# Another order of work around the chunk recurrence: the masking, the signs, the folds and tiles of the Fourier transform, and the first parts

## The reference

```python
# 1. complex recurrence per head (B=4, H=8, S=768, D=48)
scale = min(|a|, 0.999) / (|a| + 1e-6);  a_n = a * scale
for t in range(S):
    S_state = a_n[t] * S_state + outer(k[t], v[t])      # complex, k v real
    y[t]    = q[t] @ Re(S_state)
# 2. u = x + Re(FFT over channels(FFT over tokens(x))), x = y as (B, 768, 384)
#    un = layernorm(u);  x2 = u + relu(un @ w_ch1) @ w_ch2
# 3. token mixing and a second channel product on x2
```

## Time and profile before

| | us |
|---|---|
| median of 3 runs | 1131.13 (1129.0 to 1136.8) |
| the profiled execution, its own time | 1134.15 |
| its span | 1132.4 |
| TensorE busy in it | 1008.8 (89%) |
| VectorE busy | 538.2 (48%) |
| ScalarE busy | 341.4 (30%) |

### The profile page before, as it was taken

The page is one execution under the profiler, slowest core; times in us unless marked ns, Lnnn a source line. Parts: engine busy times, 40 slices in busy tenths (PEclk is TensorE's granted clock), DMA queues, the critical chain, the costliest instruction groups (busy, mean ns, idle before and its releaser), DMA issues. The chain is left out here.

```text
span 1132.4 us, 15567 instructions
## 1 busy us (share of the span) xinstructions
PE 1008.8 (89%) x6082; PEld 971.8 (86%) x6082; DVE 538.2 (48%) x1040; ACT 341.4 (30%) x515; POOL 29.9 (3%) x15
## 2 busy tenths in 40 slices
PE   0469799989969973999999999968999999999998
PEld 0348699979969863999999999968999999999998
DVE  6798877897973338332432422225223322331411
ACT  6636545655621113121122112124121220310310
POOL 0000000000000004000000000004000000000000
PEclk9859759779969895999999999999999999999999
DMA  4559777765757013602102101001001000100000
GB/s 151 150 152 301 221 226 224 208 196 156 196 145 281 22 44 100 223 29 84 33 22 69 42 28 63 15 23 43 15 8 46 24 14 21 42 21 15 6 22 21
DMA packets 96887, 104.79 MB, mean 93 GB/s; under 512 B 13121, under 2 KB 90433, under 8 KB 96834
## 3 DMA queue, kind: packets, MB, share of 16 engines
q1 hardware_dynamic: 96834, 104.07, 29.7%
HBM read 70.93 MB, written 33.11 MB: 92 GB/s over the span
## 5 line engine op out<-in xcount | busy, mean ns | idle before, releaser
L1125 ACT ACTIVATE hh<-mbank 128x384 fp32r<-128x384 f32 x192 | 94.5, 492 | 370.8 <-PE mbank L1309 370.8
L1218 DVE SCALAR_TENSOR_TENSOR hl<-mbank,hh 128x384 fp32r<-128x384 f32 x192 | 107.1, 558 | 200.9 <-ACT hh L1125 200.9
L1307 PE MATMUL mbank<-nTh,w1h 128*128 128x384 f32 x576 | 193.9, 337 | 0.7 <-DVE w1l L1240 0.7
L1308 PE MATMUL mbank<-nTl,w1h 128*128 128x384 f32 x576 | 193.2, 335 | 0.0
L1309 PE MATMUL mbank<-nTh,w1l 128*128 128x384 f32 x576 | 193.2, 335 | 0.0
L1307 PE MATMUL mbank<-w2h,hh 128*128 128x384 f32 x576 | 193.1, 335 | 0.0
L1309 PE MATMUL mbank<-w2h,hl 128*128 128x384 f32 x576 | 192.4, 334 | 0.0
L1308 PE MATMUL mbank<-w2l,hh 128*128 128x384 f32 x576 | 192.4, 334 | 0.0
L1307 PEld LDWEIGHTS mbank<-nTh,w1h 128*128 128x128 f32 x576 | 108.8, 189 | 1.5 <-issue 1.3
L1308 PEld LDWEIGHTS mbank<-nTl,w1h 128*128 128x128 f32 x576 | 108.8, 189 | 0.0
L1309 PEld LDWEIGHTS mbank<-nTh,w1l 128*128 128x128 f32 x576 | 108.7, 189 | 0.0
(11 more groups left out here) (152 smaller groups left out, 1320.7 us busy)
## 6 DMA issues: line engine op xcount, KB each, us to landing
kT<-k_turn SPq DMA_DIRECT2D x24, 384.0 KB, 3.6
qT<-q_turn SPq DMA_DIRECT2D x24, 384.0 KB, 4.4
q_turn<-w_raw SPq DMA_DIRECT2D x30, 192.0 KB, 4.4
k_turn<-t SPq DMA_DIRECT2D x24, 192.0 KB, 4.0
k_turn<-w_early SPq DMA_DIRECT2D x24, 192.0 KB, 4.6
u_scratch<-y_sb SPq DMA_DIRECT2D x24, 192.0 KB, 3.1
w_raw<-in_moe_w_ch SPq DMA_DIRECT2D x2, 2304.0 KB, 10.3
x_early<-u_scratch SPq DMA_DIRECT2D x4, 1152.0 KB, 10.0
```

Source lines behind the costliest of these rows:

```text
L1125: nc.scalar.activation(hh[:, m, :], mm_bank[(g * (KF + TPG) + m) % 2][:, 0:TG], ACT.Relu).then_inc(h_high, 1)
L1218: nc.vector.scalar_tensor_tensor(out=hl[:, m, :], in0=mm_bank[(g * (KF + TPG) + m) % 2][:, 0:TG], scalar=0.0, in1=hh[:, m, :].bitcast(fp32 ...
L1307: nc.tensor.matmul(out, lh, rh, start=(n == 0), stop=False)
L1308: nc.tensor.matmul(out, lh, rl, start=False, stop=False)
```

## The change

1. **Masking first.** `masked(m)` now stands right behind `advance_state(m-1)`, ahead of `add_transform`, folds, `phases` and `products`.
2. **Signs by ScalarE.** The two comparisons leave VectorE. `arctangents` gets two more operations of ScalarE on the whole part, Sign and Identity, and `half_angles` multiplies the arctangent by the sign. `t4` carries the offset.
3. **Products in pairs.** Chunk 0 of a part in stage 4, chunks 1 and 2 together in stage 5. SP turns chunk 0 a chunk earlier than the other two.
4. **Fourier work spread.** Before: fold, `middle` and all three widths at `j` = 1; sequence transforms 0; 1, 2; 3, 4; 5 at `j` = 2, 3, 4, 5. Now: fold 2, `middle`, width 2 at `j` = 0; folds and widths 1, 0 at `j` = 1; sequence transforms 0, 1; 2, 3; 4; 5. Tiles 0, 1 and 2, 3 are added in pairs over two banks (`f_pair`). At the very end `middle` and width 2 of block 3 stand ahead of the last `turn_y`.
5. **The smallest end** (`least`) is reduced once at the end, not per part.
6. **First parts.** `magnitudes(p0)` ahead of `squares(p1)`; the second chunk of part 1 is phased behind the products of part 0; on SP the loads for part 2 and part 3 stand ahead of `turn_decay(p0)`.
7. **ScalarE in a chunk.** `keys_turned` first, then arctangents or sines, then `evacuate_y(m-1)`, and only then squares, magnitudes or inverses and factors, then copies of widths, then `y_turned(m-1)`. Before, `evacuate_y` stood behind all of these stages.
8. `keep_busy` 3 to 4 per chunk of block 0, 6 to 5 at the start.

```diff
@@ tables of places
-            return {2: [0], 3: [1, 2], 4: [3, 4], 5: [5]}.get(j, [])
+            return {2: [0, 1], 3: [2, 3], 4: [4], 5: [5]}.get(j, [])
...
+            return [(n, i, tiles) for i, tiles in {3: [(0, 2)], 4: [(2, 2)], 5: [(4, 1)], 0: [(5, 1)]}.get(j, []) if n >= 0]
+
+        def widths_at(j):
+            return {0: [2], 1: [1, 0]}.get(j, [])
@@ SP, first parts and loop
             turn_over(0)
+            load_qk(p2)
+            load_gates(p3)
             turn_decay(p0)
-            load_gates(p3)
-            load_qk(p2)
...
                 if (m - 1, 4) in stage_at:
-                    p = stage_at[m - 1, 4]
-                    turn_over(p.first)
-                    turn_over(p.first + 1)
+                    turn_over(stage_at[m - 1, 4].first)
                 if (m - 1, 5) in stage_at:
+                    turn_over(stage_at[m - 1, 5].first + 1)
                     turn_over(stage_at[m - 1, 5].first + 2)
@@ ScalarE, arctangents and loop
+                A(im_b[p.r][:, :, T], re_b[p.r][:, :, T], ACT.Sign, scale=3.0,
+                  bias=nearly_zero[:, 0:1]).then_inc(act_step[s], 1)
+                act.wait_ge(act_step[s], act0[p.n] + 12)
+                A(t4[:, :, angles_room(p)], im_b[p.r][:, :, T], ACT.Identity, scale=-0.25,
+                  bias=quarter[:, 0:1]).then_inc(act_step[s], 1)
...
+                if j < NCH - 1:
+                    keys_turned(m)
                 if (m, 3) in stage_at:
                     arctangents(stage_at[m, 3])
                 if (m, 4) in stage_at:
                     sines(stage_at[m, 4])
-                if j < NCH - 1:
-                    keys_turned(m)
+                if m:
+                    evacuate_y(m - 1)
...
-                if m:
-                    evacuate_y(m - 1)
-                if (m, 2) in stage_at:
                     angle_tables()
-                if b and j == 1:
+                if b and j == 0:
                     middle(b - 1)
-                    for n in range(KD):
+                if b:
+                    for n in widths_at(j):
                         widths(b - 1, n)
@@ VectorE, loop
                     advance_state(m - 1)
-                for n, i in added_at(m):
-                    add_transform(n, i)
-                if b and j == 1:
-                    fold_sequence(b - 1)
+                masked(m)
+                for n, i, tiles in added_at(m):
+                    add_transform(n, i, tiles)
+                if b:
+                    for n in widths_at(j):
+                        fold_sequence(b - 1, n)
                 if (m, 3) in stage_at:
-                    phases(stage_at[m, 3])
+                    half_angles(stage_at[m, 3])
+                    phases(stage_at[m, 3], range(3))
                 if (m, 4) in stage_at:
-                    products(stage_at[m, 4], range(2))
+                    products(stage_at[m, 4], PAIRS[stage_at[m, 4].n][0:1])
                 if (m, 5) in stage_at:
-                    products(stage_at[m, 5], [2])
-                masked(m)
+                    products(stage_at[m, 5], PAIRS[stage_at[m, 5].n][1:2])
@@ TensorE, end
+            middle(B - 1)
+            width_transform(B - 1, 2)
             turn_y(NM - 1)
...
-            middle(B - 1)
-            for n in range(KD):
-                width_transform(B - 1, n)
+            width_transform(B - 1, 1)
+            width_transform(B - 1, 0)
```

More of the change, by code:

```diff
@@ L72, in recurrence_and_fourier @@
         stage_at = {(p.first - LEAD + k, k): p for p in parts[2:] for k in range(LEAD)}
-        GA = 14
-        GV = [12 + 5 * p.chunks for p in parts]
+        PAIRS = [[range(0, 1), range(1, 3)] if p.chunks == 3 else [range(p.chunks)] for p in parts]
+        GA = 16
+        GV = [10 + 3 * p.chunks + 2 * len(PAIRS[p.n]) for p in parts]
         act0 = [GA * p.turn for p in parts]
@@ L249, in _ @@
                     turn_decay(stage_at[m, 4])
-                for n, i in added_at(m - 1):
-                    store_u(n, i)
+                for n, i, tiles in added_at(m - 1):
+                    for tile in range(i, i + tiles):
+                        store_u(n, tile)
                 if m % 3 == 1:
@@ L511, in products @@
                 re, im = re_b[p.r], im_b[p.r]
-                dve.wait_ge(act_step[s], act0[p.n] + 14)
-                for i in chunks:
-                    T = slice(i * CT, (i + 1) * CT)
+                dve.wait_ge(act_step[s], act0[p.n] + 16)
+                for pair in chunks:
+                    i = pair.start
+                    T = slice(i * CT, pair.stop * CT)
                     dve.wait_ge(vec_step[s], products_done(p, i))
@@ L561, in add_transform @@
-            def add_transform(b, i):
-                n = b * NT + i
-                x = y_sb[:, n % YR, :]
-                dve.wait_ge(b_made, n + 1)
-                cc, sn = f_bank[i % 2][:, 0:FH], f_bank[i % 2][:, FH:2 * FH]
-                low, high = x[:, 0:FH], x[:, DM - 1:FH - 1:-1]
+                if n == 0:
+                    V.memset(fold[:, 1, :, 0:1], 0.0)
+                    V.tensor_copy(fold[:, 0, :, 0:1], yT[:, :, 0:1])
+                first, end = max(n * P, 1), (n + 1) * P
@@ new lines, in fold_sequence, with add_transform @@
+                fwd, back = yT[:, :, first:end], yT[:, :, S - first:S - end:-1]
+                V.tensor_tensor(fold[:, 0, :, first:end], fwd, back, ALU.add)
+                V.tensor_tensor(fold[:, 1, :, first:end], fwd, back, ALU.subtract).then_inc(folded, 1)
+            halves_added = []
+            def add_transform(b, i, tiles):
+                n, halves_done = b * NT + i, len(halves_added) + 1
+                halves_added.append(n)
+                x = y_sb[:, n % YR:n % YR + tiles, :]
+                dve.wait_ge(b_made, n + tiles)
+                f = f_pair[:, i % 2:i % 2 + tiles, :]
+                cc, sn = f[:, :, 0:FH], f[:, :, FH:2 * FH]
+                low, high = x[:, :, 0:FH], x[:, :, DM - 1:FH - 1:-1]
@@ L587, in _ @@
             scaled(p0)
+            logs(p1)
             ends(p1)
             tangents(p1)
-            phases(p0)
+            half_angles(p0)
+            phases(p0, range(1))
             scaled(p1)
-            phases(p1)
-            products(p0, range(1))
+            half_angles(p1)
+            phases(p1, range(1))
+            products(p0, PAIRS[0])
+            phases(p1, range(1, 2))
             squared(p2)
-            products(p1, range(2))
+            products(p1, PAIRS[1])
             logs(p2)
@@ L767, in _ @@
                     update(m)
-                if m < NCH:
-                    keep_busy(3)
                 if m == NCH:
                     pe.wait_ge(wide_tables_in, 5 * 16)
-                if b and j == 1:
+                if not b:
+                    keep_busy(4)
+                if b and j == 0:
                     middle(b - 1)
-                    for n in range(KD):
+                if b:
+                    for n in widths_at(j):
                         width_transform(b - 1, n)
-                if b:
                     for n in transformed_at(j):
```

144 lines of the change are left out of this document (68 added, 76 removed).

## The result

The changed kernel takes **1150.98 us** (median of 4 executions, 1150.66 to 1152.23) against 1131.91 (1129.0 to 1136.8) for the kernel before on the same chip: a ratio of 1.0166, interval 1.0129 to 1.0203. It is slower by 19 us, above the range of 1100 to 1138, where 1118.4 was forecast.

The account below looks back on a forecast made before the run. Block 0 bound by SP's queue, block 1 by a slow clock, block 2 by VectorE, block 3 by one long wait. Terms -2.0 - 0.7 + 0.9 - 7.8 - 3.1 = -12.7 gave 1118.4 us; range 1100 to 1138.

Parts of the forecast that it names:

- Six waits for additions: At `j` = 3 and 4, sequence transforms wait for paired additions behind masking: 1.4 us each, bounds 0 to 2.5.
- The wait for `yT` in chunks 12 and 18: Second half of `turn_keys` waits for ScalarE's late copy of `turn_y`: 2.8 us, once per block with preparation.
- the tail: From the last outputs to the first sequence transform: 13.5 us becomes 10.4, so -3.1; low clock may return (2 us).
- the start: Before chunk 6: 2.0 us gained, handed through SP's chain to turn 6, so -2.0; chunk 6 still waits for `kT`.
- two waits at `j` = 1: Behind sines, a table load and `magnitudes` on ScalarE, TensorE waits 2.0 us for `yT` in chunks 8 and 14.
- The wait for folds at `j` = 1: Fold late because VectorE comes from the phases of `j` = 0: 1.4 us, bounds 0 to 2.5.
- the term for the lower clock: Block 1 begins behind a wait at low clock: 6.5 us, 4.5 in its first chunk and 2 in the next.
- The sum of a block: 71 us of TensorE work plus waits gives 80.0 us: block 1 -0.7, block 2 +0.9, block 3 -7.8.
- block 1 bound by a slow clock: Chunks 6 to 11 of the kernel before: 87.2 us with TensorE at a mean clock of 0.76 of full.
- The prediction's own sign of being wrong: More than two stretches at the lower clock between chunk 8 and 418 us would show the forecast wrong.
- rival (c): ScalarE's four waits in `turn_keys` (blocks 1, 2) each bring lower clock, up to 6.5 us: +13, 1144 us; chance 0.13.

Follow-up runs that it names:

- additions first: The changed kernel with the additions of transformed tiles ahead of the masking again on VectorE: 1127.11 us, ratio 0.9932 to the kernel before.
- the filled kernel: The changed kernel with idle products of 384 columns where TensorE would wait, no wait removed: 1126.94 us, ratio 0.9943 to the kernel before.
- the second profile: The changed kernel run and profiled again, nothing altered: 1146.02 us, ratio 1.008 to the kernel before.
- both: The changed kernel with additions ahead of masking again and ScalarE's copy of the outputs back behind the stages: 1116.98 us, ratio 0.9822 to the kernel before.
- both, keys filled: The version with additions ahead of masking and the outputs' copy later, plus idle products in the key waits ahead of chunks 4 and 6: 1109.3 us, ratio 0.9775.

## Why the prediction was wrong, step by step

**Right: which waits would form, and how long.** Six waits for additions of 1.4 us were forecast ("a new wait of 1.4 us at `j` = 3, the same at `j` = 4"), and six of 1.44 to 1.45 came; a pair's additions take 2.0 us (190.09 to 192.17), as taken:

```profile
188.82 1.36 DVE L554 TENSOR_TENSOR pr<-bank,mask 128x512 f32<-128x512 f32 x2 [7.24 <-PE bank L698]
190.09 0.55 DVE L580 TENSOR_TENSOR y_sb<-y_sb,f_pair 128x386 f32<-128x386 f32 x1
190.56 0.55 DVE L581 TENSOR_TENSOR y_sb<-y_sb,f_pair 128x382 f32<-128x382 f32 x1
191.14 0.56 DVE L583 TENSOR_TENSOR y_sb<-y_sb,f_pair 128x386 f32<-128x386 f32 x1
191.61 0.55 DVE L584 TENSOR_TENSOR y_sb<-y_sb,f_pair 128x382 f32<-128x382 f32 x1
```

The wait for `yT` in chunks 12 and 18 was forecast at 2.8 and is 2.81, from the queue on ScalarE:

```profile
221.53 0.49 ACT L367 ACTIVATE y_sb<-bank 128x384 f32<-128x384 f32 x1 [4.77 <-PE bank L698]
221.92 1.15 ACT L326 ACTIVATE t<-t 128x1152 f32<-128x1152 f32 x1
223.11 1.17 ACT L328 ACTIVATE t<-t 128x1152 f32<-128x1152 f32 x1
224.18 1.15 ACT L333 ACTIVATE tok_raw<-x_early 128x1152 f32<-128x1152 f32 x1
225.36 1.16 ACT L335 ACTIVATE x_early<-x_early 128x1152 f32<-128x1152 f32 x1
226.54 1.28 ACT L389 ACT_TABLE_LOAD   x1
227.84 0.49 ACT L374 ACTIVATE yT<-bank 128x384 f32<-128x384 f32 x1
```

The table load costs 1.3 us to the next operation here too. The Trainium skill, page "ScalarE: Activation LUTs", section "What ACT_TABLE_LOAD costs", adds a drain of 1.38 us; by it this wait would have been 4.2 us, an estimate, and the trace does not agree.

The sum has this wait in the wrong blocks, though. The operations of `j` = 5 delay the first `turn_keys` of the block behind: in block 1 the wait for keys covers it, and block 3, where the sum has 0.3 us, gets 2.8.

**Right by luck: the tail.** From `middle` to the first sequence transform 417.88 - 407.67 = 10.2 us, forecast 10.4:

```profile
407.67 0.65 PE L726 MATMUL f_pair<-cd,yT 128*1 128x193 f32 x3
...
413.01 1.25 PE L740 MATMUL f_pair<-cd,fold 128*128 128x193 f32 x6 [1.58 <-DVE fold L568]
...
417.88 0.56 PE L754 MATMUL f_pair<-a_mid,tok_raw 1*128 1x193 f32 x2 [0.67 <-ACT a_sb L383]
```

The 3.1 us that were forecast are there, but not from the new order. Of the 13.5 us before, 6.8 ran at the lower level (390.5 to 397.3), which cost 3.4; none of the 10.2 did. At full clock both orders take 10.1 to 10.2 us. The terms of the forecast were 2.0 for `middle`, read at the lower level (1.1 here), and as listed they add up to 10.8, not 10.4.

**Off in size: the start.** "Still on a wait for `kT`" was right (5.81 us), -2.0 was too small: chunk 6 begins 5.7 us earlier, because turn 6 leaves at 118.48 for 124.25:

```profile
118.48 0.55 SPq L203 DMA_DIRECT2D k_turn<-t  x1
```

Turn 0 leaves at 31.12 for 34.32, 3.2 us earlier. But this is not handed down the chain: at turn 1 the lead is 0.4 us (49.12 for 49.57), at turn 3 it is 7.3, at turn 5 it is 1.1. What makes the 5.8 at turn 6 stays open. It also varies: with the same order up to there, chunk 6 begins at 130.97, 132.11, 133.59 ("additions first") and 130.95 us (the filled kernel).

**Off in place: two waits at `j` = 1.** Forecast 2.0 us in chunks 8 and 14; chunk 8 has 1.45, chunk 14 none over 0.3. This makes blocks 1 and 2 better than forecast, by 0.5 and 2 us. The wait for folds at `j` = 1, forecast at 1.4 us, is 0.8 at most.

**The step that failed: the term for the lower clock.** The sum of a block was "71 + 1.4 + 1.4 + 1.4 + 2.8 + 2.0", each wait at its length, with 6.5 us for low clock in block 1 and nothing in blocks 2 and 3. Against this stands what the trace shows (waits over 0.6 us; work is what is left when the waits and half the low time are taken off; block 3 to the first output of chunk 23):

| | forecast: work, waits, clock | measured: work, waits, clock |
|---|---|---|
| block 1 | 71, 9.0, 6.5 | 67.0, 4.3, 22.8 |
| block 2 | 71, 9.0, 0 | 67.3, 7.6, 15.4 |
| block 3 | 71, 3.1, 0 | 67.7, 5.7, 15.4 |

The clock cost 53.6 us where the sum had 6.5 (in the second profile 44.3). The work was put 11 us too high and the waits 3.5, and these errors hid part of the first: without them the miss would have been larger. Some 7 of these 11 us can be seen in the readings: `middle` and the widths took 8.2 us with the first 2.4 at the lower level (to 332.4), 1.2 us too much in each block, and six transforms were put at 2.7 where (13.2 - 8.2)/2 is 2.5, another 1.2. The rows of before had told what the clock costs: 0.76 over 87.2 us is a loss of 21 us in block 1, with no wait over 0.6 us inside it, and 0.91 and 0.90 are 7 and 9 us in the other two. The prediction called block 1 bound by a slow clock, and then priced that at 6.5 us. That this clock is at these waits and can be had back is what the filled kernels show.

The prediction's own sign of being wrong was more than two stretches at the lower clock between chunk 8 and 418 us. There are ten; the kernel before has four.

I had the mechanism as rival (c), at 0.13, with an outcome of 1144 us, near the 1146 and 1151 measured. It named the four waits in the middle of `turn_keys` only. The six for additions stand ahead of transforms of 193 columns, and neither the sum nor (c) gave them a fall; they have one each in the first profile. My reason against (c) was "the new waits are at most 3 us", beside a fall after 5.1 and 8.0 us of waiting: that longer waits bring a fall says nothing about shorter ones. And the earlier trace rows showed a fall without any wait ahead. That row said that the level can fall in this work even so, and I read it as an accident that costs 6.5 us now and then.

The Trainium skill, page "TensorE: Matmul & The Clock Gate", section "A second HAM failure mode: psum-queue depth-cycling", describes a kernel in which short idle times between groups of matmuls make the clock swing between its two levels. This trace agrees: ten waits of 1.1 to 2.8 us, and a fall at each. In the second profile one of them (283.57 us) has none.

## What to carry to other kernels

When TensorE's work is thin, do not price a wait at its length: here waits for additions cost about twice that, half of it by the lower clock. Ten short waits in place of two long ones, 5 us more in sum, made the kernel slower although VectorE had less to do. Count the waits that an edit creates, and look at the granted clock behind the ones that are there; a wait that can't be removed can be filled with idle products that end with it (1146 to 1151 us became 1127), while the same products without a wait brought nothing. Price a stretch at the clock that its own row shows: a floor read at full clock has to have the loss added back. And when a wait goes and nothing is won, look for the next one that had ended at the same time on another engine (`pr` on VectorE, `kt` on ScalarE).

## What the runs showed of the hardware that I had not expected

- The granted clock fell at waits of TensorE as short as 1.1 to 1.45 us amid narrow matmuls, and stayed down for 3.4 to 13.6 us behind these in the first profile of the changed kernel (17.1 us at the waits of 2.81). At four waits of 0.78 us there was no fall. A wait of 1.58 us between the width transforms of the tail (413.01 us above) had none either, in any of the twelve traces that have it. In "both", three of five falls between 150 and 400 us (178.6, 246.9 and 376.6 us) have no wait over 0.6 us within 3 us ahead of them.
- In "both, keys filled" only the waits ahead of chunks 4 and 6 were filled; low clock in T went from 66.2 to 20.5 us, also in blocks 2 and 3, where the kernels are the same. Whether an early fall makes later ones likelier is not shown: executions of one kernel differ as well, and this profile is of the fastest of five.
- The same program with the same waits had 107.0 us at the lower level in one profiled execution and 88.7 in another, and medians of 1150.98 and 1146.02 us.
